# Value product by groups of 128 queries in a ring of three, remainders transposed behind their tiles, every transpose taken from PSUM by ScalarE

## The reference

```python
scores = scale * np.matmul(q, k.transpose(0, 1, 3, 2))
thresh = np.max(scores, axis=-1, keepdims=True) - tau
scores = np.where(scores >= thresh, scores, -1000000000.0)
scores = scores - np.max(scores, axis=-1, keepdims=True)
attn = np.exp(scores)
attn = attn / (np.sum(attn, axis=-1, keepdims=True) + 1e-09)
out = np.matmul(attn, v)
...
h = x @ w_in; g = h - np.tanh(h); x = g @ w_out      # 2304 x 512, inner 2048
h = x @ w_in; g = h / (1.0 + np.exp(-h)); y = g @ w_out
```

## Time and profile before

| what | value |
|---|---|
| median of 3 runs | 1138.37 us (1137.86 to 1138.44) |
| the profiled execution's own time | 1138.3 us |
| its span | 1136.5 us |
| mean granted TensorE clock | 0.998 |
| busy: PE, PEld, DVE, ACT, POOL | 1107.6, 942.1, 593.3, 405.2, 263.8 us |
| value product in the attention stage ends | 343.95 us from the start |

### The profile page before, as it was taken

The page is one execution under the profiler, slowest core; times in us unless marked ns, Lnnn a source line. Parts: engine busy times, 40 slices in busy tenths (PEclk is TensorE's granted clock), DMA queues, the critical chain, the costliest instruction groups (busy, mean ns, idle before and its releaser), DMA issues.

```text
span 1136.5 us, 15338 instructions
## 1 busy us (share of the span) xinstructions
PE 1107.6 (97%) x5744; PEld 942.1 (83%) x5744; DVE 593.3 (52%) x1164; ACT 405.2 (36%) x814; POOL 263.8 (23%) x240
## 2 busy tenths in 40 slices
PE   5999999999999999999999999999999999999998
PEld 4888888888888888888888889988888888888898
DVE  7999999999966754333334334441221222221232
ACT  4787878788773221111111111242211111111111
POOL 3656656665625410000000000164100000000000
PEclk9999999999999999999999999999999999999999
DMA  6142423324023210000000000043010000000010
GB/s 157 42 117 59 111 64 87 89 60 116 17 89 115 93 56 1 1 1 0 0 0 0 0 0 1 20 130 95 17 38 1 1 37 0 0 37 0 1 38 19
DMA packets 15193, 48.46 MB, mean 43 GB/s; under 512 B 2080, under 2 KB 2592, under 8 KB 15136
## 3 DMA queue, kind: packets, MB, share of 16 engines
q1 hardware_dynamic: 15136, 47.72, 14.7%
HBM read 42.99 MB, written 4.72 MB: 42 GB/s over the span
## 4 chain that ended last, share of the span: by engine, by line
PE 73%; DVE 19%; issue 4%; ACT 0%; POOL 0%; DVEq 0%; ACTq 0%
PE hid L797 35%; PE acc L813 34%; DVE probs L571 9%; DVE stats L587 5%; DVE probs L616 5%; PE pv L715 3%; PE scores L750 1%; PE tps L776 1%; DVE x_lo L637 0%; DVE rowsum_e L580 0%; DVE rinv L609 0%; DVE pR L601 0%; ACT w_parts L470 0%; POOL q_parts L379 0%; ACT x_hi L479 0%
## 5 line engine op out<-in xcount | busy, mean ns | idle before, releaser
L797 PE MATMUL hid<-x_hi,w_parts 128*128 128x512 f32 (+1 forms) x1280 | 385.0, 368 | 2.1 <-DVE x_lo L637 2.1
L813 PE MATMUL acc<-g_hi,w_parts 128*128 128x512 f32 (+1 forms) x1280 | 384.0, 368 | 0.0
L797 PEld LDWEIGHTS hid<-x_hi,w_parts 128*128 128x128 f32 x1280 | 234.2, 189 | 42.7 <-DVE x_lo L637 2.2
L813 PEld LDWEIGHTS acc<-g_hi,w_parts 128*128 128x128 f32 x1280 | 234.1, 189 | 40.0
L797 PE MATMUL hid<-x_lo,w_parts 128*128 128x512 f32 (+1 forms) x640 | 235.4, 368 | 0.0
L813 PE MATMUL acc<-g_lo,w_parts 128*128 128x512 f32 (+1 forms) x640 | 235.4, 368 | 0.0
L651 DVE CAST g_hi<-h_act 128x512 fp32r<-128x512 f32 (+1 forms) x160 | 68.7, 429 | 271.4 <-ACT h_act L494 268.6
L392 POOL TENSOR_TENSOR w_parts<-w_raw,w_parts 128x1024 fp32r<-128x1024 f32 x30 | 73.5, 2451 | 402.0 <-ACT w_parts L470 402.0
L646 DVE TENSOR_TENSOR h_act<-hid,h_act 128x512 f32<-128x512 f32 (+1 forms) x80 | 51.1, 638 | 203.9 <-ACT h_act L491 203.9
L491 ACT ACTIVATE h_act<-hid 128x512 f32<-128x512 f32 (+1 forms) x80 | 44.4, 555 | 294.9 <-PE hid L797 294.9
L494 ACT ACTIVATE h_act<-hid 128x512 f32<-128x512 f32 (+1 forms) x80 | 44.4, 555 | 291.7 <-PE hid L797 291.7
(11 more groups left out here) (46 smaller groups left out, 815.7 us busy)
## 6 DMA issues: line engine op xcount, KB each, us to landing
w_raw<-w_in SPq DMA_DIRECT2D x32, 512.0 KB, 3.3
k_raw<-k_in SPq DMA_DIRECT2D x30, 288.0 KB, 4.9
q_raw<-q_in SPq DMA_DIRECT2D x30, 288.0 KB, 6.3
v_all<-v_in SPq DMA_DIRECT2D x16, 448.0 KB, 4.0
out<-xT SPq DMA_DIRECT2D x4, 1024.0 KB, 4.2
k_raw<-k_in SPq DMA_DIRECT2D x4, 144.0 KB, 3.0
q_raw<-q_in SPq DMA_DIRECT2D x4, 144.0 KB, 3.0
out<-xT SPq DMA_DIRECT2D x1, 512.0 KB, 2.9
```

The lines of the kernel that those rows point to most:

```text
L797: last = pe.matmul(hid[f % HBANKS][:, 0:w], a, b[:, kc, 0:w], start=(kc == 0 and i == 0), stop=(kc == KC - 1 and i == 2))
L813: last = pe.matmul(acc[n][:, 0:w], a, b[f % GRING][:, 0:w], start=(f == 0 and i == 0), stop=(f == FT - 1 and i == 2))
```

## The change

Value products go by groups instead of halves: three groups of 128 queries and one of 192 (128 and the 64 of the ninth tile), each 9 matmuls. pT and pR become rings of three such groups. The rest of a full query group is transposed in the step right behind its second tile (one block), so a pair has 14 units, all taken by ScalarE; VectorE's copy L601 is gone. ScalarE's order in a step becomes: product copy, exponential, transposes, splits (before: product copy, transposes, exponential, splits). Each of four groups is copied to xT, in phases 1, 3, 5 and 8. The queries of the next pair are split in phases 2 and 4 on ScalarE. The probabilities' buffer has 12 slots instead of 15. The first pair's next splits are no longer later than the others' (LATE_STEPS is gone). The first two weight pairs of the layers are split inside the attention stage: W_AT is step 100, the subtraction goes from VectorE to GpSimd. X_AT is step 153.

```diff
-K_STEPS = (0, 1)
-Q_STEPS = (3, 5)
-LATE_STEPS = (2, 3), (4, 5)
-UNITS = TILES + 2
+K_STEPS = (0, 1)
+Q_STEPS = (2, 4)
+UNITS = TILES + FULL + 1
+SLOTS = 12
+RINGP = 3
-L_PV = {L_S + 14: (0, 0, 2), ...
-BY_DVE = (8,)
+PV_STEPS = {0: {3: (0, 4), 4: (4, 9)}, 1: {5: (0, 4), 6: (4, 9)}, 2: {7: (0, 4), 8: (4, 9)},
+            3: {9: (0, 3), 10: (3, 6), 11: (6, 9)}}
+TAIL = NT - TILES + L_T + max(PV_STEPS[GROUPS - 1]) + 2
+W_AT = 100
+X_AT = NT + L_EXP
+H_AT = TAIL - 4
...
 # ScalarE, in a step
+                    for g, t in outputs_in(k):
+                        act.wait_ge(pv_done, GROUPS * g + t + 1)
+                        act.activation(xT[:, g % PAIRS, at:at + wide(t)], pv[:, 0:wide(t)], ...)
+                    if 0 <= n < NT:                                   # n = k - L_EXP
+                        act.activation(tile, tile, ACT.Exp, ...).then_inc(exp_done, 1)
+                    if 0 <= n < NT:                                   # n = k - L_T
+                        act.wait_ge(t_done, unit + 1)
+                        act.activation(pT[r][:, j % 2, :, 0:P], bank[:], ACT.Copy).then_inc(t_taken, 1)
...
+                        elif j % 2 == 1:
+                            act.wait_ge(t_done, unit + 1)
+                            act.activation(pR[r][:, 0:P], bank[:, 0, :], ACT.Copy).then_inc(t_taken, 1)
                     what, h = split_in(k)
...
 # TensorE, the value product
+            def product(g, t, i0, i1):
+                if i0 == 0:
+                    if G > 0:
+                        pe.wait_ge(out_taken, G)
+                for i in range(i0, i1):
+                    last = pe.matmul(pv[:, 0:w], *todo[i], start=(i == 0), stop=(i == len(todo) - 1))
...
 # VectorE, in a step
-                            dve.tensor_copy(pR[u][:, 0:FULL * P].rearrange("p (t q) -> p t q", t=FULL),
-                                            bank[:]).then_inc(t_by_dve, 1)
...
 # GpSimd
+            steps(0, W_AT)
+            weights_lo(0, 0)
+            weights_lo(0, 1)
+            steps(W_AT, TAIL)
```

More of the change, by code:

```diff
@@ L70, with place, slot_of, slot_user @@
 GRING = 3
[L73 to L82, removed]
+def place(n):
+    return divmod(n, TILES)
+def slot_of(n):
+    g, j = place(n)
+    return ((TILES + 1) * g + j) % SLOTS
+def slot_user(n):
+    g, j = place(n)
+    before, i = divmod((TILES + 1) * g + j - SLOTS, TILES + 1)
+    return before * TILES + i if before >= 0 and i < TILES else None
+def unit_of(n):
+    g, j = place(n)
+    return UNITS * g + j + j // 2
+def rest_unit(n):
+    g, j = place(n)
+    return UNITS * g + (3 * (j // 2) + 2 if j < 2 * FULL else UNITS - 1)
+def group_of(n):
+    g, j = place(n)
+    return GROUPS * g + min(j // 2, GROUPS - 1)
+def wide(t):
+    return WIDE if t == GROUPS - 1 else P
 def main_keys(j, c):
@@ L89, in main_keys, with split_in, products_in, outputs_in @@
     return slice(at, at + P)
-def split_in(k, first):
-    p, j = divmod(k, TILES)
-    if not 0 <= k < STEPS or (first and p == 0):
+def split_in(k):
+    g, j = divmod(k, TILES)
+    if not 0 < g < NPAIRS:
         return None, 0
[L98 to L102, removed]
+    if j in K_STEPS:
+        return "keys", K_STEPS.index(j)
+    if j in Q_STEPS:
+        return "queries", Q_STEPS.index(j)
     return None, 0
-def units_of(q, first):
-    p, j = divmod(q, TILES)
+def products_in(k):
     found = []
[L112 to L119, removed]
-    return found
[L123 to L144, removed]
+    for t, pieces in PV_STEPS.items():
+        for at, piece in pieces.items():
+            g, late = divmod(k - L_T - at, TILES)
+            if late == 0 and 0 <= g < NPAIRS:
+                found.append((g, t, *piece))
+    return found
+def outputs_in(k):
+    return [(g, t) for g, t, _, last in products_in(k - 1) if last == 2 * FULL + 1]
 def width(c):
     return LAST if c == CHUNKS - 1 else CHUNK
[L151 to L160, removed]
 def build(nc, q_in, k_in, v_in, tau_in, w_in, out):
@@ L348, in _, with steps @@
                                pattern=[[-1, P]], channel_multiplier=1).then_inc(consts_ready, 1)
[L350 to L359, removed]
+            def steps(k0, k1):
+                for k in range(k0, k1):
+                    n = k - L_NORM
+                    if 0 <= n < NT:
+                        if n % GROUP == 0:
+                            pool.wait_ge(rinv_done, n // GROUP + 1)
                             pool.sem_inc(pool_waited, 1)
-                        tile = probs[:, slot_of(q), :]
-                        r = rinv[:, q % RING:q % RING + 1]
+                        tile = probs[:, slot_of(n), :]
+                        r = rinv[:, n % RING:n % RING + 1]
                         pool.tensor_scalar(tile, tile, r, 1.0, ALU.mult, ALU.mult).then_inc(norm_done, 1)
-                    what, h = split_in(k - 1, first)
-                    g, u = PAIRS * B + k // TILES, k // TILES % 2
+                    what, h = split_in(k - 1)
+                    g, u = k // TILES, k // TILES % 2
                     if what == "keys":
@@ L402, in _ @@
         def _(act):
[L403 to L438, removed]
-                        n, c, tile = STEPS * B + q, q % RING, probs[:, slot_of(q), :]
@@ L779, in _, with scores_of @@
-            steps(0, range(STEPS), True)
-            for B in range(1, BATCH):
-                steps(B, range(STEPS), False)
+            def scores_of(n):
+                g, j = place(n)
+                u = g % 2
+                if n < 2:
+                    pe.wait_ge(qk_split, 2 * n + 2)
+                elif j == 0:
+                    pe.wait_ge(qk_split, 4 * g + 4)
+                if n >= SBUFS:
+                    pe.wait_ge(lift_done, n - SBUFS + 1)
+                flat = q_parts[u][:].rearrange("p h s -> p (h s)")
+                if j < 2 * FULL:
+                    at = (0 if j % 2 == 0 else 640 + REST) + j // 2 * P
+                    parts = [(j % 2, flat[:, at:at + P])]
+                else:
+                    parts = [(0, flat[:, FULL * P:FULL * P + P]), (1, flat[:, SEQ:SEQ + P])]
+                for a in range(2):
+                    todo = []
+                    for h, rows in parts:
+                        cols = [(0, a * HALF, HALF)]
+                        if h == 1 and j == 2 * FULL:
+                            cols = ([(0, REST, HALF)] if a == 0 else
+                                    [(0, HALF + REST, HALF - REST), (HALF - REST, 0, REST)])
+                        todo += [(rows, keys[:, h, k0:k0 + w], c0, w)
+                                 for keys in (k_lo[u], k_hi[u]) for c0, k0, w in cols]
+                    for i, (rows, keys, c0, w) in enumerate(todo):
+                        last = pe.matmul(scores[n % SBUFS][:, a, c0:c0 + w], rows, keys,
+                                         start=(i == 0), stop=(i == len(todo) - 1))
+                last.then_inc(scores_done, 1)
@@ new lines, in steps @@
+            def steps(k0, k1):
+                for k in range(k0, k1):
+                    if 0 <= k - L_S < NT:
+                        scores_of(k - L_S)
+                    n = k - L_T
+                    if 0 <= n < NT:
+                        j, slot = n % TILES, slot_of(n)
+                        pe.wait_ge(norm_done, n + 1)
+                        transposes(unit_of(n), [probs[:, slot, main_keys(j, c)] for c in range(FULL)])
+                        if j == 2 * FULL:
+                            transposes(rest_unit(n), [probs[:, slot, SEQ - P:SEQ]])
+                        elif j % 2 == 1:
+                            flat = probs[:].rearrange("p r s -> p (r s)")
+                            at = (slot - 1) * SEQ + FULL * P
+                            transposes(rest_unit(n), [flat[:, at:at + P]])
+                    for piece in products_in(k):
+                        product(*piece)
```

291 lines of the change are left out of this document (101 added, 190 removed).

## The result

The changed kernel takes 1147.72 us (median of 4 runs, 1146.65 to 1148.85) against 1138.34: ratio 1.0072, 95% interval 1.006 to 1.0084, so 9.4 us slower. Forecast were 1144 (+5.9) and slower. The profiled execution took 1147.15 us; its span is 1145.3, 8.8 more than before. The medians are 9.4 apart because two of the changed kernel's four executions have spans of 1146.4 and 1146.5 beside 1144.9 and 1145.3, while the four of the kernel before lie within 0.6.

A forecast was written before the change was run, and what follows sets the result against it. TensorE and VectorE shared the limit; afterwards TensorE, waiting for ScalarE, would set the pace. Start +1.1, pairs +6.0, last pair +0.3, step 100 +2.3, end -3.8: +5.9 on 1138.3, 1144 us; range 1130 to 1157.

The forecast's parts named there:

- The chain of the prediction: In a pair, `stats` of phase 1 held by GpSimd's subtraction delays ScalarE's copy of pv; TensorE waits, pair +0.46 us.
- The waits: TensorE's value products wait for ScalarE's copy of pv: 1.04 us in phase 3, 0.44 us in phase 5.
- S0: First weight load of the scores of phase 0, set to 0 as the start of the pair followed.
- S4: First weight load of the scores of phase 4, forecast at 9.17 us, after the product wait of phase 3.
- S6: First weight load of the scores of phase 6, forecast at 13.70 us, after the product wait of phase 5.
- The passes: TensorE's value passes of 128 queries were taken as 0.109 us each, loads hidden: +0.1 us a pair.
- the second rival: Weight loads show under 128-column value passes, 0.16 us each: pair 21.1 to 21.3, 1159 us; chance 0.15.
- Start: First pairs: TensorE's wait for the late split goes, but products start earlier and the second pair waits: +1.1 us.
- the end: Behind the last scores: less value work left, -4.9 us, but a product waits 1.1 behind X_AT copies: -3.8 us.
- cancelled: Rival: waits half as long, pair near 19.9 us, the total +1 us, 1139; chance 0.1.
- the faster one: Rival: `stats` of phase 1 starts ahead of the subtraction, product waits shrink, pair 19.2 us, 1130 us; chance 0.25.
- the early weights save nothing at the end: Weight splits at step 100 stall products and transposes, +2.3 us, without saving at the end, where TensorE had other work.

The follow-up runs named there:

- e1: The changed kernel with the product copies of groups 1 and 2 (phases 3 and 5) made by VectorE: 1139.76 us, ratio 1.0004 to the kernel before.
- e2: The changed kernel with the queries split in phases 3 and 5 again: 1139.3 us, ratio 1.0004 to the kernel before.
- e3: The changed kernel with GpSimd's subtraction of keys replaced by a one-input scaling (low part wrong): 1136.04 us, ratio 0.9961 to the kernel before.
- e5: The changed kernel with the first two weight pairs split at step 156 instead of step 100: 1147.31 us, ratio 1.0073 to the kernel before.
- e6: The changed kernel with VectorE's copies of groups 1 and 2 in all pairs but the last, and the weights late: 1134.88 us, ratio 0.9966.
- e9: As e6, but with the weights again at step 100: 1136.49 us, ratio 0.9983 to the kernel before.
- e11: As e6, with queries split in phases 3 and 5 and their subtraction a one-input scaling (low part wrong): 1136.64 us, ratio 0.9982.

## Why the prediction was right

**The mechanism.** The chain of the prediction (held `stats`, masked tile, exponential, take, split of queries, copy of pv, product) is what the trace shows for phase 3, link by link, and e1, e2 and e3 each cut it at another link: at the copy, at the split, at its head. Each gave 0.6 to 0.9 us a pair back.

**The waits.** Forecast 1.04 and 0.44 us, measured 0.87 and 0.63. The sum, 1.48, was measured as 1.50, but by luck: a miss of 0.17 one way and one of 0.19 the other cancel. With S0 = 0, and as the mean of six pairs, S4 and S6 came at 9.00 and 13.73, where 9.17 and 13.70 were forecast. The pair was forecast as 20.26 and is 20.43. Most of the missing 0.17 stands behind the waits, in phases 6 to 8: they were added up from passes as 6.56 and take 6.69, 0.08 of the difference in phase 8 alone, and what adds it there stays open. It is small beside what it decides: over the 12 pairs to step 136 it makes 2.0 us, of the 2.9 by which the span came out over the forecast +5.9. The medians' difference is 3.5 over it, for the reason given with the result.

**The passes.** 0.109 was taken, 0.111 measured: 54 of them make 0.1 us a pair more. A load hides under such a pass (each load lasts 0.19 in its record, and they start 0.111 apart), and the second rival (0.16 a pass) is out. The ratio that the Trainium skill gives for 128-column streams (TensorE: Matmul & The Clock Gate, Back-to-back issue gap) does not carry over to these fp32 passes; the measured pace decides.

**Once only.** Start +1.1 forecast (two steps earlier in the program), +1.6 measured (-0.6 to step 19, where -0.8 was put, and +2.2 in the second pair for +1.9); step 100 +2.3 and +2.4; the end -3.8 and -3.4, with the wait behind the tokens' copies 1.24 for 1.1. The layers did not move.

**The rivals.** Neither faster nor cancelled: the faster one needed a step of under 1.94 in phase 0, and VectorE's is 2.17 (TensorE's 2.08), so `stats` of phase 1 is held in nearly every pair. What I had not seen is how near the favourable cases were. Moving one split, or two copies, was enough for no difference to the kernel before. The statement that the early weights save nothing at the end was wrong: with late weights the end is 1.3 us longer, in e5 (19.18 for 17.85) and in e6 against e9 (19.34 for 18.02). That is less than the 2.4 and 2.7 that they cost at step 100.

**Left open.** The passes were not tried with the old halves on the changed kernel's other parts, so the price of the grouping alone, without the moved split, is known only from e2 (with it, no difference to before). Two product regions in one PSUM bank, or two banks, were not tried.

## What to carry to other kernels

Where one PSUM bank is reused, count what stands ahead of its copy on the copying engine, and ask how late the first of those operations can be. Smaller groups made the copy twice as frequent and put it behind a chain that only a timeline of one period shows, since every engine had room on average. Two moves that help apart can hurt together if both decide who starts first at a shared resource: run the combination, and look at the one step where they meet.

## What the runs showed of the hardware

A GpSimd operation with one tensor input in SBUF holds VectorE's small operation with two SBUF inputs just as one with two inputs does. The hold lasts to the end of GpSimd's operation: 170.59 and 170.58 in e3, 159.80 and 159.80 in e11. The rule of the Trainium skill (SBUF — State Buffer, Who interferes with whom), by which any reading GpSimd operation takes the pair for its whole length, agrees. I had read the rows of the kernel before as if only the subtraction did it. What starts first passes, but only if it is clearly first. In the changed kernel a `stats` started 0.17 us ahead of a subtraction and took its usual 0.22 (rows below), while the one of step 100 is listed 0.02 ahead of the subtraction of weights (218.38 and 218.40, GpSimd idle before it) and was held for all of it. In the fourteen traces the border is sharp: where GpSimd was idle, all 5 that are listed 0.00 to 0.02 ahead were held, and all 138 that are listed 0.04 or more ahead took 0.21 to 0.24. Under 0.04 us, then, the listed start does not tell who was first. In row 212.14 of the kernel before GpSimd was not idle either: its scalings, 1.46 us from 210.72 on, ended at 212.18.

```profile
207.64 0.22 DVE L549 SCALAR_TENSOR_TENSOR stats<-stat_scale,finemax,stat_bias 128x2 f32<-128x2 f32 x1
```
```profile
207.81 1.42 POOL L359 TENSOR_TENSOR q_parts<-q_raw,q_parts 64x576 fp32r<-64x576 f32 x1
```
